# A 1-core attention and two-MLP kernel: from four per-batch passes to five token chunks, with split weights kept in HBM and two heads' probabilities turned together

## What is computed

```python
scores = scale * np.matmul(q, k.transpose(0, 1, 3, 2))
kth = np.partition(scores, -top_k, axis=-1)[..., -top_k:-top_k + 1]
scores = np.where(scores >= kth, scores, -1000000000.0)
attn = np.exp(scores - np.max(scores, axis=-1, keepdims=True))
attn = attn / (np.sum(attn, axis=-1, keepdims=True) + 1e-09)
x = np.matmul(attn, v)                       # then (2304, 512)
gate = 1.0 / (1.0 + np.exp(-(x @ w_gate)))   # 512 -> 1536
y = (gate * (x @ w_val)) @ w_out             # 1536 -> 512
r = np.maximum(y @ w_in, 0.0)                # 512 -> 2048
out = (r * r) @ w_out2                       # 2048 -> 512
```

## Time and profile before

| | us |
|---|---|
| median of 3 runs (lowest, highest) | 1364.82 (1363.34, 1367.8) |
| span of the profiled execution | 1359.4 |
| the first step, attention alone | about 0 to 230 |
| three steps of attention beside an MLP | about 230 to 1140 |
| the last step, MLP alone | about 1140 to 1359 |

### The profile page before, as it was taken

How to read it: one execution, slowest core, us unless ns; L and a number is a source line. 1 busy time by engine, 2 the same in 40 slices (tenths; PEclk the granted TensorE clock), 3 DMA queues, 4 the chain that set the end, 5 groups by cost and what they waited for, 6 DMA issues and landing times.

```text
span 1359.4 us, 27024 instructions
## 1 busy us (share of the span) xinstructions
PE 1275.9 (94%) x9424; PEld 1252.3 (92%) x9424; DVE 972.7 (72%) x2032; ACT 871.6 (64%) x1764; POOL 806.8 (59%) x610
## 2 busy tenths in 40 slices
PE   3877768999999999999999999999999999999999
PEld 3767658999999999999999999999999999999998
DVE  6999996989899934989899924989899930100320
ACT  4776775877778744777778744777778742332541
POOL 4443343676577744676577744676577744663872
PEclk9976677999999999999999999999999999999999
DMA  3212020323223233333323233323223233232232
GB/s 85 70 30 50 20 49 25 84 83 85 82 77 84 76 96 102 84 82 85 85 75 90 70 89 105 88 82 85 78 82 80 78 96 88 78 94 76 80 95 73
DMA packets 49499, 105.78 MB, mean 78 GB/s; under 512 B 5968, under 2 KB 5968, under 8 KB 49360
## 3 DMA queue, kind: packets, MB, share of 16 engines
q1 hardware_dynamic: 49360, 103.99, 27.6%
HBM read 99.24 MB, written 4.72 MB: 76 GB/s over the span
## 4 chain that ended last, share of the span: by engine, by line
PE 63%; DVE 24%; issue 8%; POOL 2%; DMA 1%; ACT 1%; SPq 0%; DVEq 0%; POOLq 0%; ACTq 0%
PE ps L380 17%; PE ps L381 16%; PE ps L385 16%; DVE top L600 9%; DVE work L602 8%; PE ps L326 6%; PE ps L316 3%; DVE g_lo L656 3%; PE ps L301 3%; DVE xq L628 2%; DVE bias L597 1%; DMA raw<-qk_in 1%; POOL ring L715 1%; POOL probs L721 1%; POOL qkh L708 0%
## 5 line engine op out<-in xcount | busy, mean ns | idle before, releaser
L715 POOL TENSOR_TENSOR ring<-w_raw,ring 128x512 fp32r<-128x512 f32 x272 | 364.0, 1345 | 154.2 <-ACT ring L515 151.0
L380 PE MATMUL ps<-xy_hi,ring 128*128 128x288 f32 x1280 | 370.8, 304 | 0.7 <-ACT out_buf L497 0.7
L721 POOL TENSOR_TENSOR probs<-probs,mask 128x576 f32<-128x576 f32 x144 | 204.8, 1422 | 265.4 <-ACT mask L451 265.3
L381 PE MATMUL ps<-xy_lo,ring 128*128 128x288 f32 x1280 | 358.6, 295 | 0.0
L600 DVE MAX8 top<-work 128x8 f32<-128x576 f32 x432 | 312.1, 749 | 5.1
L385 PE MATMUL ps<-xy_hi,ring 128*128 128x288 f32 x1280 | 273.7, 295 | 0.0
L380 PE MATMUL ps<-g_hi,ring 128*128 128x288 f32 x896 | 257.9, 302 | 0.0
L381 PE MATMUL ps<-g_lo,ring 128*128 128x288 f32 x896 | 251.2, 295 | 0.0
L380 PEld LDWEIGHTS ps<-xy_hi,ring 128*128 128x128 f32 x1280 | 241.5, 189 | 1.0 <-ACT out_buf L497 1.0
L381 PEld LDWEIGHTS ps<-xy_lo,ring 128*128 128x128 f32 x1280 | 241.6, 189 | 0.0
L326 PEld LDWEIGHTS ps<-vt,probs_t 128*128 128x128 f32 x1440 | 197.5, 213 | 45.8 <-ACT probs_t L457 36.1
(11 more groups left out here) (57 smaller groups left out, 1919.1 us busy)
## 6 DMA issues: line engine op xcount, KB each, us to landing
w_raw<-w_in SPq DMA_DIRECT2D x272, 256.0 KB, 2.7
raw<-qk_in SPq DMA_DIRECT2D x68, 320.0 KB, 4.7
vt<-v_in SPq DMA_DIRECT2D x17, 325.0 KB, 5.1
out<-out_buf SPq DMA_DIRECT2D x16, 288.0 KB, 2.1
```

What stands on the lines that cost most here:

```text
L380: nc.tensor.matmul(dst, w_hi, hi[:, k, cols], start=first, stop=False)
L381: nc.tensor.matmul(dst, w_hi, lo[:, k, cols], start=False, stop=False)
L715: nc.gpsimd.tensor_tensor(out=ring[:, n % RING, 1, :], in0=w_raw[:, n % RAW, :], in1=ring[:, n % RING, 0, :].bitcast(F32), op=ALU.subtract ...
L721: nc.gpsimd.tensor_tensor(out=probs[:, t % 2, 0:SEQ], in0=probs[:, t % 2, 0:SEQ], in1=mask[:, t % 2, :], op=ALU.mult).then_inc(probs_ready, 1)
```

## The change

The kernel is written anew, with the same arithmetic of three products in the MLP.

1. **Chunks.** The 2304 tokens are taken as chunks of 320, 512, 512, 512 and 448, across the bounds of batches. An MLP product over a chunk is one matmul per weight tile and part (three instead of six), of the chunk's width, in one of three PSUM banks. Chunks cut batches, so that attention has 32 groups (a chunk's part of a batch, for a pair of heads) and 64 loads and splits of a head instead of 32.
2. **Slots.** There are 144 tiles, as before, in 148 slots with no loop: the MLP of chunk 0 begins in slot 23, of chunk 1 in 56, of 2 in 88, of 3 in 120, each beside attention of the next chunk, and that of chunk 4 stands alone after slot 147. `shares()` deals the halves out: most in slots that turn nothing.
3. **Weights.** 90 block splits remain: 23 in slots 3 to 13 (blocks 0, 3, 6, ..., before any MLP), 45 for chunk 0 and 22 for chunk 1, two of them ahead of the chunk in slots 14 and 15. SP writes both parts of each block once to `w_split` in HBM (68 stores of 512 KB), and the other 273 uses are loads of 512 KB straight into `ring`.
4. **Two heads together.** A unit is 128 queries of both heads (64 units of two tiles) or 64 queries of both (16 of one tile). ACT writes the probabilities as blocks of 64 keys of either head side by side. PE turns 9 blocks a unit and multiplies with block-diagonal values as the stationary operand; the result is already transposed, so `turn_x` is gone, and the inverses are spread by POOL (`spread_inverse`) and turned by PE to be multiplied in on POOL (`normalise`).
5. **The mask.** POOL makes bias and threshold (`bias`, 2 operations of one column), compares and scales by -2^127 (`mask`, new TENSOR_SCALAR), and adds that to the scores; ACT takes one exponential, with the sum as its by-product. The two signs on ACT, and on DVE the bias and the division, are gone; a reciprocal stays.

```diff
-            def mask_probs(b, t):
-                pool.wait_ge(exp_done, b * TILES + t + 1)
-                nc.gpsimd.tensor_tensor(out=probs[:, t % 2, 0:SEQ], in0=probs[:, t % 2, 0:SEQ],
-                                        in1=mask[:, t % 2, :], op=ALU.mult).then_inc(probs_ready, 1)
+            def mask(t):
+                pool.wait_ge(bias_done, t + 1)
+                wait(pool, exp_done, t - 1)
+                nc.gpsimd.tensor_scalar(masked[:, t % 2, :], scores[:, t % 4, :], thr[:, t % 2:t % 2 + 1], -KILL,
+                                        ALU.is_lt, ALU.mult).then_inc(mask_step, 1)
+                pool.wait_ge(mask_step, t + 1)
+                nc.gpsimd.tensor_tensor(out=masked[:, t % 2, :], in0=scores[:, t % 4, :], in1=masked[:, t % 2, :],
+                                        op=ALU.add).then_inc(mask_done, 1)
...
+            def select(t, step):
...
+                if step == 0:
+                    dve.wait_ge(s_copied, t + 1)
+                    wait(dve, bias_done, t - 1)
...
+            def load_parts(k):
+                stored = STORED_BY[JOBS[k][1]]
+                sp.wait_ge(w_stored[stored % RING], 16 * stores_to_place(stored))
+                wait_place(sp, k)
+                sp.dma_start(place(k).rearrange("p a c -> p (a c)").bitcast(F32),
+                             w_split[JOBS[k][1], :, :]).then_inc(ring_loaded[k % RING], 16)
...
+            for s in range(SLOTS):
+                if 0 <= s - MASK < NT:
+                    bias(s - MASK)
+                if s - TURN in UNIT_AT:
+                    add_eps(UNIT_AT[s - TURN])
+                if s - NORM in UNIT_AT:
+                    normalise(UNIT_AT[s - NORM])
+                if 0 <= s - MASK < NT:
+                    mask(s - MASK)
+                for c, p in X_AT.get(s, []):
+                    split_x(c, p)
+                for c, n in blocks_of(SHARES[s - 1][2]) if s else []:
+                    evac(c, n)
+                if s - TURN in UNIT_AT:
+                    spread_inverse(UNIT_AT[s - TURN])
+                for g, h in HEADS_AT.get(s, []):
+                    split_head(g, h)
+                for k in SPLIT_AT.get(s, []):
+                    split_weights(k)
+                for c, n in blocks_of(SHARES[s][0] + SHARES[s][1]):
+                    evac(c, n)
```

## The result

The changed kernel takes **1573.67 us** (median of 4, 1570.83 to 1576.41) against 1365.26 for the kernel before on the same chip: 1.153 times as long, 95% interval 1.151 to 1.155. The forecast was 1345, a little faster than before, with a range up to 1395; the kernel became slower, and by far more than that range allowed.

What follows compares the result with a forecast made beforehand. POOL was to bound chunk 0 and slow the start through DVE's waits, PE the later chunks: 171 + 228 + 774 + 164 + 3 = 1340 us of span, run time 5.4 above, about 1345; range 1255 to 1395.

Steps and rivals of the forecast that it cites:

- The comparison is not in this trace: POOL's mask comparison, once per tile, had no traced price; taken as 0.67 us, with 1.15 as the other end.
- the slope of AFFINE_SELECT: Price for POOL's comparison from 294 ns at 128 columns and 240 at 64: 0.67 us for 576.
- the square of L737: A POOL operation in the trace, taken as the other end of the comparison's price: 1.15 us.
- The bias pair: POOL's two one-column operations per tile for bias and threshold, 0.1 us each.
- the start: Slots before the first MLP matmul, with DVE waiting for POOL: 171 us, or 128 were only DVE to count.
- Chunk 0's POOL sum: POOL's work beside the MLP of chunk 0: 211 us, above PE's 184 and DVE's 181, so POOL is the bound.
- The term for POOL's waits: In 17 slots of chunk 0 POOL's wait for ACT's exponential and copy is uncovered, about 1 us: 228 in all.
- there PE stays the bound: Chunks 1 to 3: POOL has about 205 us of 264 and less after, so PE sets 774 us together.
- wrong altogether: Stated failure sign: PE waits in the middle chunks too, above all on the loop DVE, POOL, ACT.
- The clock: Rival: PE's clock falls beside chunk 0; 1380 us with half its work at 1.2 GHz, 1457 with all; chance 0.13.
- The matmul: MLP matmul of 512 columns on PE: 225 ns, from 213.3 of streaming and 12 fixed.
- the rival's 235: Rival: the MLP matmul's loss goes with its columns, 235 ns each, 1373 us in all; chance 0.15.

Runs made afterwards that it cites:

- e2_before_extra: Kernel before, with an extra 128 x 576 comparison per tile on POOL behind the product of mask and probabilities, result unused: 1486.5 us, 1.090.
- e6: Changed kernel with POOL's comparison replaced by six operation forms in turn, 24 tiles each, five without the right mask: 1526.1 us, a single run.
- e1: Changed kernel with POOL's comparison run on only 64 of the 576 columns, the others left unmasked: 1420.3 us, 1.042.
- e10: Changed kernel with comparison on 64 of 576 columns and ACT's head splits and weight copies ahead of the exponential: 1375.4 us, 1.007.
- e3: Changed kernel with four buffers instead of two for the 32 largest, so DVE waits for POOL's bias of tile t-4: 1576.6 us, 1.156.
- e5: Changed kernel with ACT's head copies and first weight copies ahead of the same slot's exponential instead of behind it: 1506.0 us, 1.105.
- e7: Changed kernel with the mask off POOL: DVE makes the bias, compares and multiplies with the exponential of raw scores: 1349.5 us, 0.990.
- e4: Changed kernel with the 273 loads of split weights cut to a quarter, 128 KB instead of 512 KB each: 1573.8 us, 1.154.
- e11: Changed kernel with the comparison on ACT, POOL subtracting, and ACT's exponential between head splits and weight copies: 1330.6 us, 0.975.
- e8: Changed kernel with the comparison on ACT, POOL subtracting, and ACT's exponential behind head splits and weight copies: 1338.1 us, 0.980.

## Why the prediction was wrong, step by step

- **The step that failed** is the sentence "The comparison is not in this trace", with what was taken for it: the slope of AFFINE_SELECT gave 0.67, the square of L737 the other end, 1.15. The operation takes 2.23 (the changed kernel, e2_before_extra and e6 agree). Both ends came from operations of another kind, and the true price was twice the upper one. The term is short by 1.56 x 144 = 225 us of POOL's work. The bias pair was sized 0.2 and takes 0.44 (66.08 to 66.52), another 35. POOL per tile is 4.2, not 2.4.
- **With the true price the method comes near in the start, and not behind it.** The start would have been 171 + 22 x 1.8 = 211 with every slot charged, and 202 with only the 17 in which the forecast had POOL set the pace; measured 215. Chunk 0's POOL sum would be 211 + 33 x 1.8 = 270 (measured 265 busy), chunk 1's 205 + 32 x 1.8 = 263 (254). But the first took 330 and the second 314. The term for POOL's waits, "about 1 us" in 17 of the slots, is the second failure: POOL stood idle 66 and 60 us in these windows. e1 and e10 test it without the dear comparison: POOL is busy 211 us in chunk 0 of both, the forecast's own figure, and the stage takes 273 in e1, with the order that the forecast assumed, and 258 in e10, not 228. So the waits are 47 to 63 us where 17 stood. Two of them from the changed kernel's chunk 0 (us in total, times, longest):

```profile
POOL xf L724 <- ACT rp L522: 26.5, 11, 4.6
...
POOL klo L669 <- ACT qkh L491: 17.8, 13, 1.9
```

  The second is of the kind that the forecast had in mind: with the weight copies (10.3) it makes 28 us there, 31 in e1 and 15 in e10. The first is of a kind that stood at nothing in the sum: POOL multiplies a unit's result with its inverses (`normalise`) ahead of the tile's mask, and so waits for PE's value products and ACT's copy of them, with the left-over units 31 us in chunk 0, 23 in e1 and in e10. No run puts `normalise` behind the mask, so what this order costs is not shown.

  The forecast's "there PE stays the bound" for chunks 1 to 3 fell with it, in the way named as wrong altogether, PE waiting there on the loop DVE, POOL, ACT. Of that loop DVE was no part that counted (e3), and PE's values, which it didn't name, may have been one.
- **The account.** From 1574.5 of span, 156 go with the comparison's length (e1, where it takes 0.15 less than the forecast's 0.67), another 44.5 with ACT's order (e10), which with the long comparison alone is worth 69 (e5). e10 is left 34 above the forecast's 1340: 30 in chunk 0, 11 in the three after it and 2 in the last, less 11 in the start.
- **The clock** did fall beside chunk 0 (0.85), along with PE's share of busy time. Where the waits shrink, it comes back: 0.90 in e1's chunk 0, 0.93 in e10's, 0.98 in e7's. PE was busy 231 of the 331 us there, so it was not the bound, and the rival as stated was not what happened. What the low clock adds by making POOL wait longer for the value products, no run separates. The argument against the rival was misread as well: the first step before has PE idle 63 of 200 us and the forecast's chunk 0 44 of 228, 1.6 times the share and not "four times as much idle".
- **The matmul** of 512 columns: 230 ns (ten distances from 1257.59 to 1259.89), between 225 and the rival's 235. A unit is 2.94 us, where 2.8 stood: nine transposes 0.90 (1250.94 to 1251.84), that of the inverses 0.11, nine value products 1.93 for 1.87. PE's timeline in chunk 3 of the changed kernel:

```profile
1255.24 0.27 PE L410 MATMUL ps<-ident,rinv_q 128*128 128x128 f32 x1
1255.35 2.17 PE L415 MATMUL ps<-pt,vt 128*128 128x128 f32 x18
1257.28 0.48 PE L456 MATMUL ps<-g_hi,ring 128*128 128x512 f32 x1
1257.59 0.39 PE L457 MATMUL ps<-g_lo,ring 128*128 128x512 f32 x1
...
1259.89 0.39 PE L458 MATMUL ps<-g_hi,ring 128*128 128x512 f32 x1
```

- **Right:** the last chunk (166 for 164), the loads hardly waited for (PE 1.8 us in all; 512 KB land in 3.5 us where 5.4 was the bound; e4), the chunks where PE is the bound (272, 254 and 255 in e11 against 270, 254 and 251), and POOL as the engine that takes the first stages' gain back, only by far more than all of it.

Of the signs that the prediction named, the MLP's first matmul came at 215 and not at 171; until then DVE had waited 83 us for `thr`, not 45 (352 in the whole span); beside chunk 0 POOL was busy 80% and not over 90, PE 70% and not 80, and the clock was 0.85, not 1.00. In e11, where the comparison is on ACT, PE is busy 88% of chunk 0 and 99% of chunk 1. Its windows of the start, chunk 0 and chunk 1:

```profile
0.00:154.00 154.00, 84.03 (x448) 74.60 (x449) 125.05 (x264) 96.53 (x186) 105.16 (x120) 0.81 0.56 195
154.00:380.00 226.00, 198.64 (x1415) 194.47 (x1413) 200.81 (x412) 155.79 (x327) 183.11 (x192) 0.97 0.60 207
380.00:651.00 271.00, 269.28 (x1524) 232.83 (x1523) 194.88 (x411) 166.87 (x329) 175.30 (x189) 1.00 0.59 206
```

## What to carry to other kernels

An operation that the trace doesn't show on that engine, and that comes once per tile, decides the forecast: bound it by the dearest row of the engine that has as many elements (here 1.51 us, L704 in the earlier trace rows, still 0.7 short), and let the range go well beyond that when the operation is of another kind. An engine in a loop of hand-overs can set the pace before it is busy all the time, here at 80%; count its waits slot by slot from the order of the queues. And one of the largest idle times in a profile may be a follower: with two more buffers 340 us of DVE's wait moved to other places and the time stayed, while a changed order on the engine that POOL waits for gave 68 us.

## What the hardware showed that I had not expected

- POOL on 128 x 576 fp32: copy 0.67 us, two-tensor operation 1.42 to 1.51, one scalar operation 1.73, two 2.16 to 2.24; between 64 and 576 columns (0.52 and 2.23 us) the slope is 3.34 ns a column. The Trainium skill (GPSIMD Engine Reference, 4.1 Engine selection) calls one-input work there roughly line-rate and two-input work the slower kind. The copy agrees with that; for scalar arithmetic these rows say the reverse, and they decide.
- A product of 2 columns on DVE takes 0.14 to 0.16 us where POOL is idle (68 of 144 in e8), and up to 1.41 beside POOL's operations with two inputs, 0.40 on the mean. Each of the 60 that take over 0.25 ends within 0.04 us of an operation of POOL, as here, at 80.25:

```profile
78.99 1.26 POOL L698 TENSOR_TENSOR ring<-w_raw,ring 128x512 fp32r<-128x512 f32 x1 [1.03 <-ACT ring L534]
79.23 1.03 DVE L631 TENSOR_TENSOR nbias<-top,factors 128x2 f32<-128x2 f32 x1
```

  So a small operation of DVE paid for POOL's, by some 37 us in e8's 144 tiles. The Trainium skill (SBUF — State Buffer, SBUF: two separate sides) tells of a port pair that a DVE operation with two inputs and a GpSimd operation take in turn, for the whole instruction; these rows agree with it.
- The exponential's sum as a by-product is a separate ACT operation of 0.19 to 0.20 us behind it (ACTIVATION_READ_ACCUMULATOR in the changed kernel and in e8).
